# A recurrence woven into an MLP on one Trainium2 core: its window stages spread over ten slots instead of seven

## The reference

```python
for t in range(S):
    cur = einsum('bhd,bhe->bhde', u[None] * k[t], v[t])
    y[t] = einsum('bhd,bhde->bhe', r[t], state + cur)
    state = w[t][..., None] * state + einsum('bhd,bhe->bhde', k[t], v[t])
x = y.transpose(0, 2, 1, 3).reshape(3072, 384)
h = x @ w_in                                   # 384 x 2048
g = where(h >= 1, h, where(h <= -1, 0, (h + 1)**2 / 4))
x = g @ w_out                                  # 2048 x 384
g, val = x @ w_gate, x @ w_val                 # 384 x 1536
out = (silu(g) * val) @ w_out2                 # 1536 x 384
```

## Time and profile before

| | |
|---|---|
| median of 3 runs | 1028.84 us |
| the profiled execution, its own time | 1028.84 us |
| its span in the trace | 1027.0 us |
| granted TensorE clock, mean | 0.993 |
| PE busy | 976.9 us, 95% |
| PE weight loads busy | 957.2 us, 93% |
| DVE busy | 556.4 us, 54% |
| ACT busy | 395.8 us, 39% |
| POOL busy | 131.6 us, 13% |
| chain that ended last | PE 91%, DVE 5% |

### The profile page before, as it was taken

How to read it: one execution, slowest core, us unless ns; L and a number is a source line. 1 busy time by engine, 2 the same in 40 slices (tenths; PEclk the granted TensorE clock), 3 DMA queues, 4 the chain that set the end, 5 groups by cost and what they waited for, 6 DMA issues and landing times.

```text
span 1027.0 us, 17262 instructions
## 1 busy us (share of the span) xinstructions
PE 976.9 (95%) x6874; PEld 957.2 (93%) x6874; DVE 556.4 (54%) x978; ACT 395.8 (39%) x799; POOL 131.6 (13%) x90
## 2 busy tenths in 40 slices
PE   1488999999999999999999999999999999999997
PEld 0478999999999999999999999999999999999997
DVE  7956686776857768676444443333333343433332
ACT  3444445454454544544476422222222222222211
POOL 3741030200302003020045400000000000000000
PEclk9989999999999999999999999999999999999999
DMA  7461040411304123040132401010000101010000
GB/s 227 140 201 28 18 157 1 147 28 40 135 1 146 28 57 119 1 147 2 55 101 86 130 1 47 1 47 1 14 32 0 46 0 46 0 46 0 23 1 25
DMA packets 23203, 59.72 MB, mean 58 GB/s; under 512 B 2656, under 2 KB 11488, under 8 KB 23136
## 3 DMA queue, kind: packets, MB, share of 16 engines
q1 hardware_dynamic: 23136, 58.79, 17.8%
HBM read 49.34 MB, written 9.44 MB: 57 GB/s over the span
## 4 chain that ended last, share of the span: by engine, by line
PE 91%; DVE 5%; issue 1%; ACT 1%; DMA 1%; SPq 0%; DVEq 0%; ACTq 0%
PE bank L1047 49%; PE bank L1071 34%; PE bank L1097 2%; PE bank L1119 2%; PE bank L1114 1%; PE bank L1090 1%; PE bank L1107 1%; PE bank L1125 1%; DVE w_by_channel L847 1%; DVE k_by_channel L856 1%; DVE w_window L839 1%; DVE suf L834 1%; DVE r_by_channel L864 0%; DMA w_by_channel<-in_w_channel 0%; DMA ring<-in_w_in 0%
## 5 line engine op out<-in xcount | busy, mean ns | idle before, releaser
L923 DVE TENSOR_TENSOR glo<-gate,ghi 128x384 fp32r<-128x384 f32 x224 | 136.4, 609 | 122.9 <-ACT ghi L694 122.9
L694 ACT ACTIVATE ghi<-gate 128x384 fp32r<-128x384 f32 x224 | 117.4, 524 | 207.7 <-DVE gate L942 95.4
L940 DVE TENSOR_TENSOR gate<-bank,gate 128x384 f32<-128x384 f32 x96 | 53.6, 558 | 221.7 <-ACT gate L798 221.7
L1047 PE MATMUL bank<-xlo,w2gv_ahi 128*128 128x384 f32 x480 | 162.1, 338 | 0.0
L1047 PE MATMUL bank<-xhi,w2gv_alo 128*128 128x384 f32 x480 | 162.1, 338 | 0.0
L1047 PE MATMUL bank<-xhi,w2gv_ahi 128*128 128x384 f32 x480 | 162.1, 338 | 0.0
L798 ACT ACTIVATE gate<-bank 128x384 f32<-128x384 f32 x96 | 47.3, 493 | 234.4 <-PE bank L1047 234.4
L1071 PE MATMUL bank<-ghi,w1ohi 128*128 128x384 f32 x384 | 134.5, 350 | 3.3 <-DVE glo L923 3.2
L1047 PE MATMUL bank<-xhi,w1ihi 128*128 128x384 f32 x384 | 131.2, 342 | 1.3 <-DVE xlo L918 1.3
L1047 PE MATMUL bank<-xlo,w1ihi 128*128 128x384 f32 x384 | 131.0, 341 | 0.0
L1047 PE MATMUL bank<-xhi,w1ilo 128*128 128x384 f32 x384 | 130.9, 341 | 0.0
(11 more groups left out here) (81 smaller groups left out, 1544.8 us busy)
## 6 DMA issues: line engine op xcount, KB each, us to landing
w_by_channel<-in_w_channel SPq DMA_DIRECT2D x16, 339.5 KB, 4.0
k_by_channel<-in_k_channel SPq DMA_DIRECT2D x16, 336.0 KB, 4.9
r_by_channel<-in_r_channel SPq DMA_DIRECT2D x16, 336.0 KB, 5.5
ring<-in_w_out SPq DMA_DIRECT2D x28, 192.0 KB, 2.7
r_k_diag<-in_r_token SPq DMA_DIRECT2D x8, 576.0 KB, 7.1
k_by_token<-in_k_token SPq DMA_DIRECT2D x8, 576.0 KB, 8.3
v_by_token<-in_v_token SPq DMA_DIRECT2D x8, 576.0 KB, 9.2
x_t<-ring SPq DMA_DIRECT2D x8, 576.0 KB, 3.0
```

What stands on the lines that cost most here:

```text
L694: e.activation(ghi[j % 2][:, :], gate[j % 2][:, :], ACT.Copy).then_inc(M["hi", ph], 1)
L923: e.tensor_tensor(glo[j % 2][:, :], gate[j % 2][:, :], ghi[j % 2][:, :].bitcast(F32), ALU.subtract)\
L940: e.tensor_tensor(q, hid[j % 2][:, 0:T], q, ALU.mult).then_inc(M["t", 2], 1)
L1047: m = e.matmul(out, w_of(a, k), x_of(b_, k), start=start and i == 0, stop=stop and i == total - 1)
```

## The change

The list `FILLS` is written flat, and in it KT of the next window stands ahead of Y of this one, where before it stood behind. The fills now stand two to a slot from slot 3 on: (KT0, AT0 0), (AT0 1, ST0), (KT1, Y0), (AT1 0, AT1 1), (XT0, ST1), (KT2, Y1), (AT2 0, AT2 1), (XT1, ST2) in slots 3 to 10, then Y2 in slot 11 and XT2 in slot 12, as before. The scans move from slots 7, 10, 13, 14 to 10, 12, 13, 14. All else is as it was.

```diff
-VISITS = [[("KT", 0, 0), ("AT", 0, 0), ("AT", 0, 1)],
-          [("ST", 0, 0), ("Y", 0, 0), ("KT", 1, 0)],
-          [("AT", 1, 0), ("AT", 1, 1), ("XT", 0, 0)],
-          [("ST", 1, 0), ("Y", 1, 0), ("KT", 2, 0)],
-          [("AT", 2, 0), ("AT", 2, 1), ("XT", 1, 0)],
-          [("ST", 2, 0), ("Y", 2, 0)],
-          [("XT", 2, 0)]]
-FILLS = [f for visit in VISITS for f in visit]
+FILLS = [("KT", 0, 0), ("AT", 0, 0), ("AT", 0, 1), ("ST", 0, 0), ("KT", 1, 0), ("Y", 0, 0),
+         ("AT", 1, 0), ("AT", 1, 1), ("XT", 0, 0), ("ST", 1, 0), ("KT", 2, 0), ("Y", 1, 0),
+         ("AT", 2, 0), ("AT", 2, 1), ("XT", 1, 0), ("ST", 2, 0), ("Y", 2, 0), ("XT", 2, 0)]
...
-WIN_SLOTS = {j: tuple(FILLS.index(f) for f in visit) for j, visit in zip((3, 5, 6, 8, 9, 11, 12), VISITS)}
+WIN_SLOTS = {3 + i: (2 * i, 2 * i + 1) for i in range(NF // 2)}
+WIN_SLOTS[11], WIN_SLOTS[12] = (NF - 2,), (NF - 1,)
...
-SCAN_SLOTS = {7: 0, 10: 1, 13: 2, 14: 3}
+SCAN_SLOTS = {10: 0, 12: 1, 13: 2, 14: 3}
```

## The result

The changed kernel takes 1038.46 us (median of 4 runs, 1037.47 to 1039.87) against 1028.16 us before on the same chip (median of 4, 1027.15 to 1029.99). The ratio is 1.0099, 95% interval 1.008 to 1.0118, that is 8.2 to 12.1 us slower. The profiled execution took 1037.86 us with a span of 1036.1 us, 9.1 us more than the span before.

The account below looks back on a forecast made before the run. The prediction took PE's own instruction stream to bound phase 1, since PE hardly waits there. It added 6.7 us for new narrow blocks and 1.4 for moved transposes, 8.1 us on 1028.84, to get 1036.9 us, range 1032 to 1041.

Parts of the forecast that it names:

- The split: ST parted from Y in phase 1: three more narrow blocks a group, 21 at 0.32 us, 6.7 us more on PE.
- The price taken from a block of two one-column matmuls: Stepping from wide matmuls into narrow ones and back costs PE 0.32 us, read at a lone check in the last group.
- way in of 0.09 us: Going from the last wide matmul into a narrow block takes PE 0.09 us over the ordinary pitch.
- The transposes: KT and XT no longer follow Y and AT; four ways out a group lead to wide matmuls, costing 1.4 us.
- The waits of the fills: New distances between fills and DVE's reads in phase 1 are covered by wide matmuls; costed at nothing.
- The scans: Added scan in slot 12 delays DVE, absorbed by its idle time in slot 0; 0, bounds -0 and +2 us.
- rival 3: DVE falls behind from slot 10 to slot 0, PE waits for `glo` in slot 2; 1039 to 1047 us, chance 0.10.
- The prologue: Swapped fills run while PE waits for DVE anyway, end set by a weight load; 0, bounds -1.5 and +1 us.
- The sum: Block and transpose costs on PE together: 8.1 us slower, on 1028.84 us, giving 1036.9 us.
- Rival 1: Steps into narrow blocks are free in phase 1, nine blocks cost what six do; 1028.8 us, chance 0.10.
- rival 2: Prologue shortens as KT1 and KT2 run in PE's idle time, up to 5 us; 1023.8 us, chance 0.03.

Follow-up runs that it names:

- experiment 1: Kernel before with ST standing alone in slots 4, 7 and 10, the rest of the fills and the scans as before; 1036.86 us, ratio 1.007.
- experiment 5: Kernel before with 21 added one-column, one-row matmuls, each alone between wide matmuls; 1034.17 us, ratio 1.0057.
- experiment 8: Kernel before with its fills regrouped into five narrow blocks a group instead of six, in ten slots instead of seven; 1030.09 us, ratio 1.0014.
- experiment 2: Kernel before with KT of the next window put ahead of Y, in the same seven visits, scans as before; 1032.29 us, ratio 1.0033.
- experiment 3: Kernel before with only the scans moved, to slots 10, 12, 13, 14; 1028.88 us, ratio 1.0002.
- experiment 10: Changed kernel with the scaling of one head pair on DVE moved from slot 0 to slot 1; 1034.23 us, ratio 1.005 against before.
- experiment 4: Changed kernel with the scans put back to slots 7, 10, 13, 14; 1036.38 us, ratio 1.0072 against before.
- experiment 9: Kernel before with the scaling of one head pair on DVE moved from slot 0 to slot 1; 1026.45 us, ratio 0.9981.

## Why the prediction was right

*The split, 6.7 us predicted.* Shown: 0.98 us a group, 6.9 us, in the trace of experiment 1, and 5.8 to 8.5 us by time. The price taken from a block of two one-column matmuls held for all three new ones, and experiment 5 reproduces it with no work in the block. ST and Y both use a stationary of 64 columns; experiment 8 shows that it is not a price for every pair of fills. The prediction has the new blocks stand between wide matmuls. Four of them in fact stand behind transposes (ST behind XT, Y behind KT, two each), and that the price is the same there was assumed, not read; experiment 2 bears it out. Its reading of the weight loads was short, too: it says that the trace goes against the overlap of load and matmul only where the running matmul is narrow, but its own way in of 0.09 us has a wide matmul running.

*The transposes, 1.4 us predicted.* Shown: 13.51 against 13.34 a group, 0.17, 1.2 us. Experiment 2 shows that this term is small only because the split had already been paid: alone the swap costs 4.5 us.

*The waits of the fills, 0.* Right: no wait of PE for a bank, att or ST behind the prologue.

*The scans, 0 with +2 as bound.* Too low. The step said that the lateness of about 0.3 us is absorbed where DVE idles 0.66 us. DVE was indeed left with 0.48 us of idle time, but behind it POOL holds DVE up, and `lo` of slot 2 had hardly anything to spare before; with the third scan POOL's product ends later, 1.06 us into the group instead of 0.88 in the quiet groups, and `lo` ends 0.42 behind it. The three kernels with the new scans show this (after, experiments 3 and 10), those with the old ones don't (before, experiments 1, 2, 4 and 9). Why the product ends later was not traced. The lateness reached PE as 0.13 to 0.15 us over the shortest time of 7.90 in groups 1, 2, 5 and 6. For all six groups that makes an estimate of 0.8 us for the scans. The 0.46 us by which group 4 is longer than before goes with a product that starts late there (1.33 us ahead of the group, before 1.84); experiments 1, 2 and 4, with the old scans, take 8.05 to 8.39 us there, so it is not shown to be the scans'. This is the start of rival 3. Idle time on an engine is not slack if the work behind it has a deadline.

*The prologue, 0.* Right (0.2 us), by the mechanism named: the wait moved from the state to y.

*The sum.* 8.1 us predicted; span 9.1, of which 8.1 blocks and 0.9 slots 1 and 2; median 10.3, interval 8.2 to 12.1. The 1.2 us between span and median were not traced. The median of before that this uses, 1028.16 from four runs, is low: the three sets of experiments, 20 to 23 runs of before in each and each on a chip of its own, gave 1028.69 to 1028.97, against which the changed kernel's median is 9.5 to 9.8 us longer. Rival 1 is excluded by experiments 1, 5 and 10, rival 2 by the prologue's end.

## What to carry to other kernels

On a saturated TensorE, count the places where the stream changes between full wide matmuls and small partial ones, and measure one such place between starts, not by busy time: here it cost 0.3 us, between wide matmuls and beside transposes alike. Keep small matmuls of the same tile shape together, and spread them only if an engine behind them really makes TensorE wait. And look at the waits that every version shares: moving the scaling of one head pair on DVE behind a deadline gained 2 us where the fills' order had none to give.

## What the runs showed of the hardware that was not expected

- A matmul with a stationary of 128x128 took 0.11 us with 16 columns as with 128 (0.22 us for two, both times; 0.12 for one).
- Entering a partial stationary (128x1, 128x64, 48x128) from a full one took 0.09 us over the pitch; entering 112x128 or 128x128 took nothing. Joining two different partial forms saved 0.18 to 0.20 of 0.31 to 0.32 us.
- A DVE operation of 0.53 us (two inputs in SBUF) took 2.60 when it started 0.5 us behind a POOL product of 2.68 us. It ended 0.42 us after the product. The same operation lasted from 1.36 to 2.70 us in the 66 groups looked at and ended 0.40 to 0.43 us after the product in every one: that fits an operation held until POOL is done, and not one that runs slower throughout.
- In slices 2 and 3 of the 40 the granted clock was 0.6 and 0.7 of full in the changed kernel and 0.9 and 0.8 before, with phase 1 starting within 0.2 us. The record does not go with the pace of PE: from the first of AT's 16 matmuls to the start of the next fill it is 2.01 us before (at 51.79, granted clock 1.00 from 44 to 58 us) and 2.01 us after (at 50.66, granted clock 0.56), where phase 1 has 1.09. So this difference in the record had no price.
